# One block for both phases, a later wait for the last state's move, and a split remainder around the first gather

## The reference

```python
for t in range(S):                                  # per batch and head
    S_re, S_im = ar * S_re - ai * S_im + kv, ar * S_im + ai * S_re
    y[:, :, t] = q[:, :, t] @ S_re
x = y as (3072 tokens, 384)
h = x @ w_in;  g = max(h, 0) + alpha * min(h, 0);  x = g @ w_out      # d_ff 2048
compute = x @ w_skip > 0                            # other tokens pass through
e = argmax(x @ w_gate);  weight = softmax(x @ w_gate)[e]
out = x + weight * (max(x @ w1[e], 0) @ w2[e])      # 8 experts, width 1024
```

## Time and profile before

| | us |
|---|---|
| median of 3 runs (855.49 to 857.2) | 857.11 |
| profiled execution, own time | 853.47 |
| its span in the trace | 851.5 |
| PE busy in the span | 718.7 |
| DVE busy | 607.5 |
| ACT busy | 478.3 |
| GpSimd busy | 54.7 |

### The profile page before, as it was taken

One profiled execution on the slowest core, in us unless ns is written; L12 is line 12 of the kernel. 1 busy time (PEld: TensorE's weight loads), 2 busy tenths in 40 slices (PEclk: granted clock), 3 DMA queues, 4 the chain that ended last, 5 costly groups with the idle time before them and its releaser, 6 DMA issues. The chain is left out here.

```text
span 851.5 us, 15352 instructions
## 1 busy us (share of the span) xinstructions
PE 718.7 (84%) x5454; PEld 693.5 (81%) x5454; DVE 607.5 (71%) x1250; ACT 478.3 (56%) x937; POOL 54.7 (6%) x56
## 2 busy tenths in 40 slices
PE   1213749999999999999999999999989639899895
PEld 1213749999999999999999999999889539799895
DVE  4986978997997997998899799654333454344442
ACT  8267369479559739937946964843423243233320
POOL 2000000000000000000000000000000122223222
PEclk9998769999999999999999999999989859899999
DMA  5465553345145325515515523442600376914200
GB/s 166 155 204 119 148 153 98 75 121 175 45 122 172 90 60 172 145 48 146 175 34 145 159 74 77 131 121 58 212 26 1 116 278 225 318 39 171 95 27 20
DMA packets 82429, 104.67 MB, mean 123 GB/s; under 512 B 15990, under 2 KB 68384, under 8 KB 82336
## 3 DMA queue, kind: packets, MB, share of 16 engines
q1 hardware_dynamic: 79648, 98.44, 38.9%
q0 software_dynamic: 1792, 3.76, 1.4%
q10 hardware_dynamic: 896, 1.25, 0.6%
HBM read 61.04 MB, written 12.19 MB: 86 GB/s over the span
## 5 line engine op out<-in xcount | busy, mean ns | idle before, releaser
L658 PE MATMUL out_ps<-w_out_hi,g_parts 128*128 128x394 f32 x768 | 219.8, 347 | 0.0
L646 PE MATMUL mlp_ps<-xT,w_in_hi 128*128 128x384 f32 x768 | 205.0, 349 | 14.8 <-DVE g L1493 13.9
L646 PEld LDWEIGHTS mlp_ps<-xT,w_in_hi 128*128 128x128 f32 x768 | 139.4, 192 | 21.7 <-DVE g L1493 19.7
L658 PEld LDWEIGHTS out_ps<-w_out_hi,g_parts 128*128 128x128 f32 x768 | 142.0, 188 | 2.6 <-issue 1.8
L646 PE MATMUL mlp_ps<-xT,w_in_lo 128*128 128x384 f32 x384 | 131.2, 342 | 0.0
L658 PE MATMUL out_ps<-w_out_lo,g_parts 128*128 128x394 f32 x384 | 131.0, 341 | 0.0
L1493 DVE SCALAR_TENSOR_TENSOR g<-mlp_ps,slope_side,bent 128x384 f32<-128x384 f32 x128 | 77.8, 613 | 67.7 <-ACT bent L964 59.4
L964 ACT ACTIVATE bent<-mlp_ps,bend_size 128x384 f32<-128x384 f32 x128 | 73.8, 577 | 92.0 <-PE mlp_ps L646 91.9
L972 ACT ACTIVATE g_parts<-g 128x384 fp32r<-128x384 f32 x128 | 66.2, 517 | 56.7 <-PE out_ps L658 49.7
L2279 ACT ACTIVATE hT<-mlp_ps 128x256 fp32r<-128x256 f32 x52 | 20.0, 384 | 100.2 <-PE mlp_ps L2210 100.2
L646 PEld LDWEIGHTS mlp_ps<-xT,w_in_lo 128*128 128x128 f32 x384 | 73.6, 192 | 0.0
(11 more groups left out here) (163 smaller groups left out, 1212.8 us busy)
## 6 DMA issues: line engine op xcount, KB each, us to landing
kq<-qk_dec SPq DMA_DIRECT2D x88, 144.0 KB, 3.0
arena<-in_a SPq DMA_DIRECT2D x24, 384.0 KB, 4.3
arena<-in_qk SPq DMA_DIRECT2D x24, 384.0 KB, 3.4
w_sb<-in_w SPq DMA_DIRECT2D x6, 1536.0 KB, 8.1
w_raw<-in_w SPq DMA_DIRECT2D x6, 1536.0 KB, 11.8
xT<-y_parts SPq DMA_DIRECT2D x48, 144.0 KB, 2.8
arena<-in_w SPq DMA_DIRECT2D x4, 1536.0 KB, 8.9
v_nat<-in_v SPq DMA_DIRECT2D x24, 192.0 KB, 3.9
```

The lines of the kernel that those rows point to most:

```text
L646: last = pe.matmul(ps[:, 0:HT], w_in_v[s][:, kk, f * P:(f + 1) * P], xT[n.p][:, kk, m, :], start=(kk == 0 and j == 0), stop=(kk == KT - 1 ...
L658: last = pe.matmul(out_ps[i][:, 0:DL], g_parts[:, f % 4, s, i * P:(i + 1) * P], w_out_v[m][:, f, :], start=(f == 0 and j == 0), stop=(f == ...
```

## The change

- Both phases are in one block, so the barrier between them is gone. The semaphores of phase 2 get names that begin with `routed_` and live beside those of phase 1.
- What the barrier guarded is now guarded by semaphores: DVE's first instruction of phase 2 waits for `logits_taken` (3), GpSimd's first for the last `down` (`g_used`). ACT's `take_last` copies all three logits before the three copies of the channels.
- DVE's wait for the last state's move stands behind the last half's pairs.
- ACT rounds `w2` of expert 0 right after the exponential, ahead of the table's late rows. DVE makes its remainder in two halves of 1536 elements: one before it waits for the table, one after the first slot's rows have come and were copied (`keep_x(1)`).
- GpSimd's first gather waits for the first of the two address copies alone.

```diff
@@ build
+        block = ctx.enter_context(nc.Block())
+        g_used, logits_taken = phase1(nc, qk, v, a, mask_in, w_in, w_pack, alpha, w_skip, w_gate, w1, w2, out, x2_rows,
+               mlp_ps, out_ps, att_ps, ident, logits, arena, rows, x2_stored, first_loaded, sem, block)
+        phase2(nc, w1, w2, out, x2_rows, mlp_ps, out_ps, att_ps, ident, logits, arena, rows, x2_stored, first_loaded,
+               sem, block, g_used, logits_taken)
@@ phase1, before @block.sync
-        block = ctx.enter_context(nc.Block())
@@ phase1, @block.scalar
+            def take_last(n):
+                act.wait_ge(g_used, val(n.n * NF + (NF + 4)))
+                act.wait_ge(x2_stored, val(n.n * 32 + 1))
+                first = (n.n * NC).value()
+                for i in range(NC):
+                    act.activation(logits[:, bass.ds(first + i, 1), :].rearrange("p a l -> p (a l)"),
+                                   out_ps[i][:, DM:DM + LANES], ACT.Copy).then_inc(logits_taken, 1)
+                for i in range(NC):
+                    act.activation(x2[:, i, 0:DM], out_ps[i][:, 0:DM], ACT.Copy).then_inc(x2_taken, 1)
...
-            take_x2(last_n)
+            take_last(last_n)
@@ phase1, @block.vector
             last_n = Half(0, HALVES - 1)
-            dve.wait_ge(state_moved, NC * HALVES * 64)
             for f in range(NF + 1):
                 pair(last_n, f)
-
+            dve.wait_ge(state_moved, NC * HALVES * 64)
@@ phase2, @block.scalar
             act.wait_ge(diff_made, 1)
             act.activation(expd[:, :, :], diff[:, :, :], ACT.Exp).then_inc(exp_made, 1)
+            split(0)
             act.wait_ge(rows_known, 1)
...
-            split(0)
             split(1)
@@ phase2, @block.vector
+            dve.wait_ge(logits_taken, NC)
             dve.tensor_scalar(dropped[:, :], skip, 0.0, BIG, ALU.is_le, ALU.mult).then_inc(skips_placed, 1)
...
+            def split_half(part):
+                f = slice(part * NFE // 2, (part + 1) * NFE // 2)
+                return dve.tensor_tensor(w2_v[0][1][:, f, :], w2_raw[0][:, f, :], w2_v[0][0][:, f, :].bitcast(F32), ALU.subtract)
+
+            dve.wait_ge(w2_hi, 1)
+            split_half(0).then_inc(half_split, 1)
             dve.wait_ge(table_full, 1)
...
             dve.tensor_copy(scatter_at[:, :], tab[:, NSLOT - 1, 0:1]).then_inc(first_at, 1)
-            split(0)
             dve.wait_ge(slots_known, 1)
             slots_here = slots_of_all(dve)
             keep_x(1)
+            dve.wait_ge(half_split, 1)
+            split_half(1).then_inc(w2_lo, 1)
@@ phase2, @block.gpsimd
+            pool.wait_ge(g_used, HALVES * NF + 4)
             pool.sem_inc(b_done, 1)
...
             pool.wait_ge(pads_made, 1)
+            pool.wait_ge(first_at, 1)
+            gather()
             pool.wait_ge(first_at, 2)
-            gather()
             pool.memset(y[:, :], 0.0).then_inc(pads_made, 1)
```

More of the change, by code:

```diff
@@ L132, in build @@
         first_loaded = [sem(f"first_loaded{i}") for i in range(2)]
-        phase1(nc, qk, v, a, mask_in, w_in, w_pack, alpha, w_skip, w_gate, w1, w2, out, x2_rows,
-               mlp_ps, out_ps, att_ps, ident, logits, arena, rows, x2_stored, first_loaded)
-        phase2(nc, w1, w2, out, x2_rows, mlp_ps, out_ps, att_ps, ident, logits, arena, rows, x2_stored, first_loaded)
+        block = ctx.enter_context(nc.Block())
[3 more added lines that the diff above has]
+               sem, block, g_used, logits_taken)
 def phase1(nc, qk, v, a, mask_in, w_in, w_pack, alpha, w_skip, w_gate, w1, w2, out, x2_rows,
-           mlp_ps, out_ps, att_ps, ident, logits, arena, rows, x2_stored, first_loaded):
+           mlp_ps, out_ps, att_ps, ident, logits, arena, rows, x2_stored, first_loaded, sem, block):
     with ExitStack() as ctx:
-        def sem(name):
-            return ctx.enter_context(nc.semaphore(name))
         def sb(name, shape, dt=F32):
@@ L253, in phase1 @@
         x2_taken = sem("x2_taken")
+        logits_taken = sem("logits_taken")
         def att(h, name, c):
@@ L1990, in _, with phase2 @@
                                pattern=[[-1, P]], channel_multiplier=1).then_inc(consts, 1)
-def phase2(nc, w1, w2, out, x2_rows, mlp_ps, out_ps, att_ps, ident, logits, arena, rows, x2_stored, first_loaded):
+        return g_used, logits_taken
+def phase2(nc, w1, w2, out, x2_rows, mlp_ps, out_ps, att_ps, ident, logits, arena, rows, x2_stored, first_loaded,
+           kernel_sem, block, g_used, logits_taken):
     with ExitStack() as ctx:
         def sem(name):
-            return ctx.enter_context(nc.semaphore(name))
+            return kernel_sem(f"routed_{name}")
         def sb(name, shape, dt=F32):
@@ L2093, in phase2 @@
         w2_lo = sem("w2_lo")
+        half_split = sem("half_split")
         expert_left = sem("expert_left")
@@ L2239, in _, with split @@
         def _(act):
+            def split(e):
+                p = e % BODY
+                if e >= BODY:
+                    act.wait_ge(expert_left, e - BODY + 1)
+                act.wait_ge(w2_loaded[p], e // BODY * 16 + 16)
+                act.activation(w2_v[p][0][:, :, :], w2_raw[p][:, :, :], ACT.Copy).then_inc(w2_hi, 1)
             act.wait_ge(diff_made, 1)
             act.activation(expd[:, :, :], diff[:, :, :], ACT.Exp).then_inc(exp_made, 1)
+            split(0)
             act.wait_ge(rows_known, 1)
```

## The result

| | before | changed |
|---|---|---|
| median of 4 runs each, us | 856.3 | 843.62 |
| lowest and highest | 854.88 to 857.2 | 841.58 to 845.22 |
| profiled execution's span | 851.5 | 842.8 |

The ratio is 0.9852 with a 95% interval of 0.9822 to 0.9882, 12.7 us less. Beside later experiments the changed kernel was run once more: 843.09 us against 853.35, ratio 0.9876 (0.9852 to 0.99), 10.3 us less. The forecast was 11.7 us. Each ratio is taken to runs of the kernel before that were made beside it, whose median was 856.3 us in the one set and 853.35 in the other; so kernels of different sets are compared through their ratios.

What follows compares the result with a forecast made beforehand. PE was taken as the bound, busy 718.7 of 851.5 us, with time to gain where it stands still or runs at its lower clock. Gains of 7.6 + 4.1 = 11.7 us from 857.11 gave 845.4 us, range 842.0 to 849.5.

Steps and rivals of the forecast that it cites:

- A: Start of the last half's MLP: moving the state's wait removes PE's idle and lower clock, 7.6 us gained.
- C: Table and first gather: the gather's instruction takes 1.01 instead of 3.31 us; with the border, 4.1 us gained.
- rival of a wait kept at the half's start: Last half's start: PE waits for `g` as in earlier halves; 9.7 us gained in all, 847.4 us, chance 0.12.
- B: Border between the phases: DVE begins to route once the three logits copies are there, 2.4 us earlier.
- rival of a late ACT: Border: ACT's instructions after its branch come late, 2.4 us of gain go; 9.3 us stay, 847.8 us, chance 0.06.
- under 1 us: Ranking matmuls after the border: shorter PE idling may let them find the full clock, gaining under 1 us, later lost.
- untouched gather: First gather: DMA engines take its packets between the loads'; 4.8 us for border and gather, 844.7 us, chance 0.12.
- held gather: First gather: weight loads delay its landing; 1.3 us for border and gather, 848.2 us, chance 0.12.
- The second half of the remainder: Second gather: overlaps its instruction by about 0.3 us; counted as nothing, 0.3 us without the cover of 48 cold matmuls.
- slower rival: Expert stage: code arrives late at seven changes of expert, 17.8 us more, 863.2 us; decided from 21.8 us, chance 0.03.

Runs made afterwards that it cites:

- e1: Kernel before with only DVE's wait for the last state's move put behind the last half's pairs: 846.49 us against 852.78, ratio 0.993.
- e3: Changed kernel with expert 0's remainder whole again, behind the address copies: 843.58 us, ratio to the kernel before 0.99.
- e6: Changed kernel with logits and channels copied by turns again, DVE still waiting for the logits alone: ratio to the kernel before 0.9865.
- e4: Changed kernel with expert 2's weight loads sent behind the first gather: ratio to the kernel before 0.9876.
- e7: Changed kernel with the loads of experts 2 and 3 behind the second gather and expert 0's remainder whole: 842.45 us, ratio to the kernel before 0.9878.
- e10: Changed kernel with expert 2's loads behind the first gather, later loads held until the fifth landed, remainder whole: 841.67 us, ratio to the kernel before 0.9875.
- e0: Changed kernel run once more, unaltered: 843.09 us against 853.35 for the kernel before, ratio 0.9876.
- e11: Kernel before run once more, unaltered, for a second profile: ratio to itself 1.0001.
- e8: Changed kernel with the loads from expert 4's w1 on held until the fifth gather has landed: 839.86 us, ratio to the kernel before 0.9834.
- e5: Changed kernel with the loads of experts 2 and 3 behind the second gather: 843.5 us, ratio to the kernel before 0.9884.

## Why the prediction was right

The forecast was 845.4 us and 11.7 us of gain; 843.62 us, 12.7 us and, in another set of runs, 10.3 us were measured. The stages that the edit changes give 7.9 + 3.2 = 11.1 us. That this is so near 11.7 is in part luck: A gave 0.3 us more than predicted and C 0.9 less. What the measured 12.7 has beyond the stages is no effect of the change that the runs can show.

*A, the state's wait.* Predicted 7.6 us, with 8.0 as the bound. The half took 48.99 to 49.05 us in all eleven profiles with the later wait and 56.18 to 56.97 in the three without: 7.1 to 8.0 us. By the time of e1 alone it is 6.0 us (4.4 to 7.4). The third `up` began with no gap. The rival of a wait kept at the half's start is out: PE had none there.

*B, the border.* Predicted 2.4 us, measured 2.5 (3.25 to 0.72). ACT's exponential started at 669.89 and was done 0.9 us before DVE's `total` read it at 671.22, so the rival of a late ACT is out. PE's ranking matmuls sometimes found the full clock (2.90 us of idle ahead of them, granted clock 1.00 in the changed kernel's execution) and sometimes not (0.50 in e3); that moves the table by 0.7 us, as "under 1 us" said, and by e6 none of it reaches the transposes.

*C, table and gather.* This is the term that was mis-sized. For B and C together I took 4.1 us, by a landing 0.9 us behind the old edge of the loads. It was 3.2 to 3.3 us. The instruction shrank as predicted, to 1.20 us. But from its end to the transposes it took 4.4 us, and not about 3. The landing came 1.1 us after the edge, and the edge itself, measured from the last `down`, moved from 22.8 to 23.4 us. That fits the gather's own bytes being ahead of it now (an estimate: 128 rows of 1.5 KB at the 380 GB/s of these stretches are 0.5 us). The untouched gather, 4.8 us, is out, and with it the use of the round-robin rule of "DMA: Bandwidth & Descriptors" (section on queues, rings and completion order) in the Trainium skill for this: under full weight loads the gather took 4.4 us from its descriptors to PE, in e4 2.1. The engines may well go round between queues, but that doesn't make the gather free. The held gather, 1.3 us for B and C, is out as well, since the loads end soon.

What I had not seen is what this means for the edit. If the end of the loads sets the landing, the shorter instruction and the 0.7 us of the logits' order are covered. e6 shows it for the order, at 24.41 us. For the halves e3 shows it but for the 0.74 us that its table came late, and e7 and e10 with 24.46 us and the whole remainder. So of the 3.2 us nothing that these stages can tell belongs to the halves: the opened border brings the gather up to the edge of the loads, and there it stops.

*The second half of the remainder.* It did run in the second gather's way. The gather's instruction took 1.19 us (1.01 before), 7.5 us to its landing where it was 6.6, and PE waited 0.62 us for it. I had priced this at nothing, 0.3 without its cover. That wait can't be put down to the second half, though: in e3, without it, the second gather took 1.01 us and 7.3 to its landing, and PE waited 0.23. PE came for the rows sooner, because its 48 matmuls before took 7.08 us (7.31 in e3, 7.80 before); in e0, where they took 8.09, it didn't wait. So the landing comes late under the loads in any case, and the cover that I relied on is thin.

*The experts' code.* The waits came to 8.7 us where they were 10.1, and to 9.2 in e0 and 9.1 in e11. The slower rival, a sum over 21.8 us, never came near. What it rests on does show, though: at the second change of expert the wait is 3.3 to 4.3 us in all kernels with the loads in the old place, and 0.7 to 1.5 in e7 to e10, where no loads are in flight there.

## What to carry to other kernels

Before an engine starts a stage it is worth asking for each thing it waits for who reads the result: here 7 to 8 of the 11 us that the changed stages gained came from a wait for a move that nobody read, a third of it through the clock that PE lost while it stood. When an edit shortens the making of a transfer, look at what else is in the DMA engines at its new time; if they are full, the transfer ends with the load, and the order of the loads is the thing to change. Weights that are prefetched early compete with small transfers on the chain and, as it seems, with the program's own code.

## What the runs showed of the hardware

GpSimd's indirect gather of 128 rows takes 1.0 to 1.2 us when DVE does nothing, and 3.3 to 3.4 us beside DVE's remainder of 3072 elements, which itself takes 3.35 us. In "SBUF — State Buffer" (section on the two separate sides) the Trainium skill says that a DVE operation with two inputs in SBUF can take, for its whole length, the port pair that it shares with GpSimd, against a GpSimd operation that reads SBUF, and that the other is then fully blocked. The remainder has two inputs in SBUF and the gather reads its addresses from there; the trace agrees. In the earlier trace rows the remainder ends at 695.75 and the gather's instruction 1.07 us later, at 696.82. Beside a half of 1536 elements (1.75 us, e4's second gather) the instruction takes 1.66 us and ends 0.88 us after the half: it looks as if it began only when DVE was done.

PE's waits for nothing that the profile shows, where it goes from one expert's code to the next, were 0.6 to 2.0 us at a mean DMA share of up to 0.40 in the wait, and 2.1 to 4.3 us where loads were under way beside the wait or just before it, at shares of 0.29 to 1.06 (e7: 1.10 at 0.00, 2.12 at 1.05; e8: 1.46 at 0.00; e4: 2.62 at 0.29). That it is the code that arrives late is an inference from the place and the load; no run moved the code alone.

PE's clock, after 2.9 us of idle, was granted at 1.00 in the changed kernel's ranking matmuls and at 0.50 in e3's, with the same program up to there. In the expert stage 48 matmuls took 5.62 us after 2.38 us of idling in e5, and 7.25 us after 2.12 us in e7 (granted clock 0.59 in their first 2 us). The first phase reaches its last half at a time that scatters by 8.0 us over the eleven profiles with one block and by 4.6 us over the three with two. What in its first part does that was not tried.
